# Layer 3 by Strassen's seven products over a pair of batches, in a float32r kernel of attention and two gated layers

## The reference, cut to what matters

```
x = attention(x, state)                        # 8 batches of 512 tokens and 32 states: rows of 512
x = ((x @ w1) * (x @ w2)) @ w3 @ w_out         # first stage, 4352 rows, d_ff 1024
h = x @ w_in                                   # second stage, layer 3: [rows, 512] @ [512, 2048]
g = h - tanh(h)
out = g @ w_out2                               # layer 4: [rows, 2048] @ [2048, 512]
```

## Time and profile before

| what | value |
|---|---|
| median of 3 runs | 1243.88 us (1243.76 to 1244.55) |
| profiled execution | span 1242.0 us, first to last instruction; the median of the runs is 1.9 us above it |
| TensorE (PE) | busy 1235.9 us, 6628 matmul records |
| VectorE (DVE), ScalarE (ACT) | busy 801.1 us (64%) and 547.7 us (44%) |
| DMA | 63.95 MB, mean 51 GB/s |
| stages | layer 3 begins at 492.6 us |

### The profile page before, as it was taken

The page is one execution under the profiler, slowest core; times in us unless marked ns, Lnnn a source line. Parts: engine busy times, 40 slices in busy tenths (PEclk is TensorE's granted clock), DMA queues, the critical chain, the costliest instruction groups (busy, mean ns, idle before and its releaser), DMA issues.

```text
span 1242.0 us, 16996 instructions
## 1 busy us (share of the span) xinstructions
PE 1235.9 (100%) x6628; PEld 1003.7 (81%) x6628; DVE 801.1 (64%) x1298; ACT 547.7 (44%) x1027; POOL 1.3 (0%) x7
## 2 busy tenths in 40 slices
PE   9999999999999999999999999999999999999998
PEld 6789777777777778888888888888888888888887
DVE  4666566555455435888677677676676776766776
ACT  6663334333333334545444444444444344444444
POOL 0000000000000000000000000000000000000000
PEclk9999999999999999999999999999999999999999
DMA  9932000000000120311101001001001001010000
GB/s 375 403 121 77 9 35 8 28 34 1 35 35 1 68 88 32 98 55 35 51 18 49 3 18 51 1 18 51 1 17 51 9 9 51 18 43 1 9 35 18
DMA packets 17786, 63.95 MB, mean 51 GB/s; under 512 B 1984, under 2 KB 3520, under 8 KB 13104
## 3 DMA queue, kind: packets, MB, share of 16 engines
q1 hardware_dynamic: 16976, 62.00, 13.7%
q10 hardware_dynamic: 704, 0.85, 0.2%
q0 software_dynamic: 32, 0.07, 0.0%
HBM read 45.09 MB, written 17.83 MB: 51 GB/s over the span
## 4 chain that ended last, share of the span: by engine, by line
issue 100%; POOLq 0%; POOL 0%
POOLq L261 0%; POOL ident L440 0%; POOL ident L438 0%; POOLq L440 0%; POOLq L1495 0%
## 5 line engine op out<-in xcount | busy, mean ns | idle before, releaser
L1273 ACT ACTIVATE hq<-bank 128x512 f32<-128x512 f32 (+1 forms) x144 | 82.7, 575 | 394.7 <-PE bank L1408 394.7
L1344 DVE TENSOR_TENSOR hw<-hw,hq 128x512 f32<-128x512 f32 (+1 forms) x144 | 95.5, 663 | 192.2 <-ACT hw L1284 191.9
L1408 PE MATMUL bank<-ysp_hi,wi_hi 128*128 128x512 f32 (+1 forms) x576 | 217.4, 377 | 0.0
L1408 PE MATMUL bank<-ysp_hi,wi_lo 128*128 128x512 f32 (+1 forms) x576 | 217.3, 377 | 0.0
L1408 PE MATMUL bank<-ysp_lo,wi_hi 128*128 128x512 f32 (+1 forms) x576 | 217.2, 377 | 0.0
L1435 PE MATMUL wide<-wz_hi,gsp_hi 128*128 128x512 f32 x544 | 212.3, 390 | 0.0
L1435 PE MATMUL wide<-wz_lo,gsp_hi 128*128 128x512 f32 x544 | 211.8, 389 | 0.0
L1435 PE MATMUL wide<-wz_hi,gsp_lo 128*128 128x512 f32 x544 | 211.7, 389 | 0.0
L1408 PEld LDWEIGHTS bank<-ysp_hi,wi_hi 128*128 128x128 f32 x576 | 108.3, 188 | 21.4 <-DVE gb L1363 0.9
L1408 PEld LDWEIGHTS bank<-ysp_lo,wi_hi 128*128 128x128 f32 x576 | 108.4, 188 | 20.4
L1408 PEld LDWEIGHTS bank<-ysp_hi,wi_lo 128*128 128x128 f32 x576 | 108.2, 188 | 19.9
(11 more groups left out here) (123 smaller groups left out, 1739.1 us busy)
## 6 DMA issues: line engine op xcount, KB each, us to landing
xT<-in_x_cols SPq DMA_DIRECT2D x8, 1024.0 KB, 8.6
xs<-in_x_rows SPq DMA_DIRECT2D x8, 1024.0 KB, 8.3
y_dram<-ysb SPq DMA_DIRECT2D x8, 1024.0 KB, 3.8
out<-ysb SPq DMA_DIRECT2D x8, 1024.0 KB, 4.6
yr<-y_dram SPq DMA_DIRECT2D x28, 256.0 KB, 4.1
w_raw<-in_moe_w SPq DMA_DIRECT2D x8, 512.0 KB, 10.8
wi_raw<-in_moe_w_in SPq DMA_DIRECT2D x4, 1024.0 KB, 7.6
raw<-in_moe_w_out SPq DMA_DIRECT2D x16, 256.0 KB, 2.6
```

Source lines behind the costliest of these rows:

```text
L1273: act.activation(hq[:, f % 2, 0:w], ph[f % 2][:, 0:w], ACT.Square).then_inc(sq_done, 1)
L1344: dve.tensor_tensor(u, u, q, ALU.mult).then_inc(w2_done, 1)
L1408: mm = pe.matmul(ph[f % 2][:, 0:w], wi[s][c][:, f * P:(f + 1) * P], ysp[k][u][c][:, 0:w], start=c + m == 0, stop=c == KC - 1 and m == LAST)
```

## The change

Only the second stage's first layer and what follows from it is changed; the front and the first stage's own layers compute as before.

**Seven products.** Two batches are taken together (pair i, tiles 2i and 2i+1), and two blocks of hidden columns (step p, 0 to 7). With w_in cut in four by inner half and by block (A11 to A22) and y cut in four by inner half and by batch (B11 to B22), the four blocks of h come from seven products in Winograd's form instead of eight. A product is 2 parts x 3 passes = 6 matmuls. Sums of A (S1 to S4) and of B (T1 to T4) are split into hi and lo like the blocks themselves. The products run in two PSUM banks, `acc` and `diff`, and three times an intermediate sum is copied out by ScalarE (`snap`) before the bank is gone on with.

**Weights by way of DRAM.** During the first stage `Pieces` loads w_in and w_out2, makes the four sums, splits everything and stores it to `wi_parts` and `wz_parts` in DRAM. In the second stage each step's seven split pieces (1.75 MB) are loaded anew into one of two slots, and each w_out2 block (0.5 MB) for each tile into one of six.

**Order.** In a step TensorE runs the seven products and, in four halves of 6 matmuls, two layer-4 blocks of the pair's first tile. g of the second tile (`g2`) is held in SBUF; its layer 4 runs after the eight steps, in `phase` and `other`, in the banks that the products used, and its last blocks go on into the next pair's step 0 (`column`). The states' tile runs inside that phase of the last pair, with w_in blocks from DRAM and without Strassen. The comparison `far` moves from VectorE to ScalarE (a Relu with a steep slope), and elementwise work is done 1024 wide, two blocks at once.

The core of the diff:

```diff
+    def load_wi(self, sp, n):
+        if n >= 2:
+            sp.wait_ge(self.p4_done, n - 1)
+            sp.wait_ge(self.p2_done, n - 1)
+        sp.dma_start(plain(self.wi[n % 2][:, :, :, :, :].rearrange("p s o k c -> p s o (k c)")), self.pieces.wi_parts[n % NP, :, :, 1:NOPS, :]
+                     ).then_inc(self.wi_in[n % 2], 16)
...
+    def product(self, pe, i, p, to, op, at, start, done):
+        n = NP * i + p
+        if p == 0:
+            pe.wait_ge(self.ysp_lo, NY * i + Y_ORDER.index(at) + 1)
+        wi = self.wi[n % 2]
+        for k in range(2):
+            for m, (s, t) in enumerate(PASSES):
+                mm = pe.matmul(to, wi[:, s, op - 1, k, :], (self.y_hi, self.y_lo)[t][:, at, k, :], start=start and k + m == 0,
+                               stop=k == 1 and m == LAST, skip_group_check=not start)
+        mm.then_inc(done, 1)
...
+    def p7(self, pe, i, p):
+        pe.wait_ge(self.su2_done, NP * i + p + 1)
+        self.product(pe, i, p, self.acc, S3, T3, False, self.p7_done)
...
+        def step(i, p):
+            n = NP * i + p
+            far2(n - 1)
+            if p == 1:
+                copy_s1(n)
+                copy_s5(n)
+            else:
+                copy_s5(n)
+                copy_s1(n)
+            high1(n - 1)
+            tanh2(n - 1)
+            copy_su2(n)
+            if p == NP - 1:
+                high2(i, 0)
+            square1(n)
+            far1(n)
+            tanh1(n)
+            copy_c21(n)
+            square2(n)
...
+        def first_step(i):
+            n = NP * i
+            add_c12(n)
+            if i == 0:
+                after_first(dve)
+            add_c22(n)
+            add_c11(n)
+        def step(i, p):
+            n = NP * i + p
+            poly1(n - 1, BOTH)
+            near1(n - 1, BOTH)
+            select1(n - 1, BOTH)
+            rest1(n - 1, BOTH)
+            poly2(n - 1)
+            low1(n - 1)
+            add_c12(n)
+            near2(n - 1)
+            add_c22(n)
+            select2(n - 1)
+            rest2(n - 1)
+            add_c11(n)
...
+        def first_step(i):
+            opening(i)
+            if i == 0:
+                finish(pe, range(2))
             else:
+                column(i - 1, 2, TAIL)
+            second.p6(pe, i, 0)
+            second.p3(pe, i, 0)
+            if i > 0:
+                column(i - 1, 3, TAIL[:2])
+            second.p7(pe, i, 0)
+            if i == 0:
+                finish(pe, range(2, KC))
             else:
+                column(i - 1, 3, TAIL[2:])
+            second.p4(pe, i, 0)
+            second.p2(pe, i, 0)
...
+        def step(i, p):
+            if p == 1:
+                second.p1(pe, i, p)
+                second.p5(pe, i, p)
+            else:
+                second.p5(pe, i, p)
+                second.p1(pe, i, p)
+                first(i, 2 * p - 3, 0)
+            second.p6(pe, i, p)
+            second.p3(pe, i, p)
+            if p > 1:
+                first(i, 2 * p - 3, 1)
+            second.p7(pe, i, p)
+            second.p2(pe, i, p)
+            first(i, 2 * p - 2, 0)
+            second.p4(pe, i, p)
+            first(i, 2 * p - 2, 1)
+        def phase(i):
+            first(i, 13)
+            for f in range(2):
+                block(i, 1, f, (0, 1))
+            first(i, 14)
+            first(i, 15)
+            for f in range(2):
+                block(i, 1, f, (2, 3)).then_inc(l4_second, 1)
...
+        for i in range(PAIRS):
+            at = 2 * NF2 * i
+            last = i == PAIRS - 1
+            for p in range(NP):
+                n = NP * i + p
+                load_wz(at + 2 * p + 3)
+                if n + 2 < NP * PAIRS:
+                    second.load_wi(sp, n + 2)
+                else:
+                    load_states_wi(n + 2 - NP * PAIRS)
+                if p == NP - 1 and not last:
+                    second.load_y(sp, i + 1)
+                load_wz(at + 2 * p + 4)
+                if p == 1 and i > 0:
+                    store_second(i - 1)
+            if not last:
+                load_wz(at + 19)
+                store_first(i)
+                for r in range(20, 2 * NF2 + 3):
+                    load_wz(at + r)
...
-                mm = pe.matmul(ph[f % 2][:, 0:w], wi[s][c][:, f * P:(f + 1) * P], ysp[k][u][c][:, 0:w],
-                               start=c + m == 0, stop=c == KC - 1 and m == LAST)
```

More of the change, by code:

```diff
@@ L74 @@
 WRING = 3
+NP = NF2 // 2
+NOPS = 8
+A21, A11, A12, A22, S1, S2, S3, S4 = range(NOPS)
+NY = 7
+B11, B21, B22, T1, T2, T3, T4 = range(NY)
+Y_ORDER = (T1, B11, T2, B22, T3, B21, T4)
+WZ = 6
+USES = [(0, f) for f in range(14)] + [(1, 0), (1, 1), (0, 14), (0, 15)] + [(1, f) for f in range(2, NF2)]
+NEAR, C3, C5 = 3.5 / 64, -1.0 / 3.0, 2.0 / 15.0
+ROOT = C5 ** 0.25
+KAPPA = C3 / C5 ** 0.5
+STEEP = 1e10
 class Map:
@@ L247, in build @@
-        y_hi, y_lo, y_out = sem("y2_hi"), sem("y2_lo"), sem("y_out")
-        y_copied = [sem("y_copied0"), sem("y_copied1")]
[L249 to L254, removed]
+        cut, cut_ready = small("cut", [P, 1]), sem("cut_ready")
+        l2_done, y_out = sem("l2_done"), sem("y_out")
@@ L258, in build @@
[L258 to L259 removed]
+                          w34, y_dram, s1_done, pieces, second, bank)
+        moe2 = stage_moe2(nc, sem, base, w_at, moe1["l1_done"], l2_done, y_copied, ys_out, y_out, second, pieces, y_dram, out, bank)
         with nc.Block("stages") as block:
@@ L1029, in entry, with layer2, tensor @@
                         rows.vector_back(dve, b + 2)
[L1030 to L1043 removed]
+                if not last:
+                    prepare(b, f)
+                elif f == 0:
+                    pieces.vector_half(dve, B - 1, 1)
+                elif f == 3:
+                    for n in (0, 1):
+                        second.vector_ysum(dve, 0, n)
+                elif f == 4:
+                    for n in (2, 3):
+                        second.vector_ysum(dve, 0, n)
+                elif f == 5:
+                    for n in (0, 1):
+                        second.vector_ysplit(dve, 0, n)
+                elif f == 6:
+                    for n in (2, 3):
+                        second.vector_ysplit(dve, 0, n)
+                elif f == 7:
+                    for n in (4, 5, 6):
+                        second.vector_ysplit(dve, 0, n)
+        for b in range(B):
+            entry(b, b % 2, last=b == B - 1)
+    def layer2(pe, b, f, cols=range(KC)):
+        n = NF1 * b + f
+        pe.wait_ge(p_lo, n + 1)
+        if f == 0:
+            if b == 0:
+                pe.wait_ge(ys_copied, KC)
+            for k in range(2):
+                after(pe, y_copied[k], 2 * b)
+        for c in cols:
+            for m, (s, t) in enumerate(PASSES):
+                mm = pe.matmul(py[c], w34[s][:, f, c * P:(c + 1) * P], psp[t][:, f % 2, :],
+                               start=f + m == 0, stop=f == NF1 - 1 and m == LAST)
+            if c == KC - 1:
+                mm.then_inc(l2_done, 1)
+    def tensor(pe):
         def layer1(b, f, k, last):
```

1215 lines of the change are left out of this document (827 added, 388 removed).

## The result

| | before | changed |
|---|---|---|
| median | 1243.82 us (1243.71 to 1244.55, 4 runs) | 1227.00 us (1225.78 to 1227.53, 4 runs) |
| profiled execution | span 1242.0 us | span 1223.9 us |

The ratio is 0.9862, 95% interval 0.985 to 0.9874: 16.8 us faster, where 23.2 were forecast (1220.7). In the profiled execution the granted clock was 1.00; in the other three runs it was 0.997 or 0.998 and the spans 1.0 to 1.8 us longer.

The account below looks back on a forecast made before the run. TensorE, fed all the time, was taken as the bound, so only fewer or faster matmuls help. -43.5 + 12.4 + 2.3 + 2.0 + 3.6 = -23.2: span 1242.0 to 1218.8, median 1220.7 us, range 1209 to 1240.

Parts of the forecast that it names:

- What goes: Layer 3 of the eight tiles: 192 of 1536 matmuls go, 0.227 us each, -43.5 us.
- A full step: Steps 2 to 7: VectorE's 12.8 us fit in TensorE's 14.96, P7 has 1.7 us to spare, nothing added.
- Step 1: Step 1 of each pair: TensorE stands 3.1 us at P6 and P7, four times, +12.4 us.
- Pair 0's P4: Pair 0, step 0: P4 waits for c22, which VectorE issues behind `after_first`, +2.3 us.
- Transition and transfers: Steps to phase: two level arrivals per pair, +2.0 us; second tile's block f = 4 late behind the store, +3.6 us.
- place (a): Loads at the end of the steps: landed at 26.5 at 407 GB/s, last needed at 28.6, priced 0.
- the rule: Trainium skill's HBM rate for one core, about 358 GB/s; by it place (a) lands at about 28.1, still in time.
- First stage: Work that `Pieces` adds to VectorE and ScalarE is covered by TensorE, 0; upper end +1.2 x 7.
- rival 1: Transfers late in every phase, by in-order queue waits or 322 GB/s or less: +8 to +20, 1229 to 1241; chance 0.14.
- rival 2: Hand-over chain before P7 decides every step: at +1.5 per step +36, 1257 us; chance 0.06.
- rival 3: Clock falls after step 1's waits: 30 matmuls per pair at 1.2 GHz, +24, 1245 us; chance 0.06.
- Rivals 4 (no change) and 5 (less would be paid): TensorE waits elsewhere, within 2.5 us of 1243.9, chance 0.04; step 1's waits half as long, late block hidden, 1211, chance 0.08.

Follow-up runs that it names:

- experiment 6: Changed kernel with product P7 done twice in steps 1 to 7 of each pair, 168 matmuls more: 1264.74 us.
- experiment 5: Changed kernel with two more 1024-column copies on ScalarE ahead of su2 in steps 3 to 7: 1239.21 us.
- experiment 2: Changed kernel with ScalarE's copies s1 and s5 ahead of far2, su2 right behind it, in step 1 of each pair: 1224.40 us.
- experiment 4: Changed kernel with VectorE's addition c22 of the very first step ahead of the copies of the last tile's y: 1223.60 us.
- experiment 1: Changed kernel with the second tile's w_out2 blocks f = 4 and 5 issued ahead of the 1 MB store, pairs 0 to 2: 1220.31 us.
- experiment 7: Changed kernel with the edits of experiments 1, 2 and 4 together: 1215.06 us.
- experiment 8: Changed kernel with experiments 1 and 4, experiment 3's order in step 1, and half w_out2 blocks ahead of P5 and P6 in step 2: 1212.88 us.
- experiment 3: Experiment 2 plus VectorE's order in step 1: c12 ahead of poly2 and low1, c22 right behind low1: 1230.78 us, changed kernel 1227.00.

## Why the prediction was right, and where it was off

The direction, the mechanism and the range (1209 to 1240) held; the time was 6.3 us too low. Of its four signs of being wrong two came, both in small: layer 3 starts at 493.4 us (the sign said later than 493), and the clock was under 1.00 in three of four executions. The other two did not: no full step is over 14.96 us, and releases by DMA add up to 6.5 us, not 10. By the steps of the prediction:

- **What goes, -43.5.** Right. 1344 matmuls, and 0.225 us for each that was added again (experiment 6).
- **A full step, 0.** Right: 14.96 us in every one. The spare in front of P7 was 1.4 us, not 1.7 (experiment 5).
- **Step 1, +12.4.** 13.8: 3.4 in pairs 1 to 3, where SyncE's loads over steps 1 and 2 are 29.20 us apart and the matmuls need 25.84, and 3.7 in pair 0, where two copies of y (L1108, 1.07 us) stand in ScalarE's queue ahead of them too. Cause right: moving the copies in ScalarE's queue moves the waits (experiment 2). Undersized by the spacing of dependent wide instructions on VectorE, 1.31 and 1.42 instead of 1.25 and 1.30.
- **Pair 0's P4, +2.3.** 2.25, and it goes with one line moved (experiment 4).
- **Transition and transfers, +2.0 and +3.6.** Together 10.4. This is the step that failed, in size. The late blocks cost 2.2 us and not 1.2 in each of three phases. Counted from the start of the last step (613.70 - 14.96 = 598.74) the store is issued at 30.0 and not 29.6, and the block is there at 36.4 and not 35.5: store and block one after the other take 6.4 us, not 5.9. Small waits add 0.5 a phase, as forecast. And the last pair's 2.1 us were not foreseen: 1.2 of them is the states' third layer 3, whose megabyte is only asked for when its buffer is free, at 1144.2, and is there 9.3 us later. For block f = 4 the rate was no part of it: the same bytes in the same window, four blocks of them ahead of the store, made no wait (experiment 1). But place (a), priced at 0, was not free. In pair 1 (last step from 768.10) block f = 2, issued ahead of the store and behind the pieces and the next y, was there after 29.4 us and not 26.5, and was due at 28.6. TensorE waited 0.6 for it. That made the phase no longer, since block f = 4 came no later for it; with f = 4's wait gone, 0.2 us in one phase stay (experiment 7). The first row below is of TensorE; the second is a window, with the DMA engines full (1.00):

```profile
797.60 1.63 PE L1981 MATMUL bank<-wz,gsp 128*128 128x512 f32 x6 [0.56 <-DMA wz<-wz_parts]
```

```profile
785.00:790.00 5.00, 5.00 (x23) 3.88 (x22) 4.93 (x7) 2.29 (x3) 0.00 (x0) 1.00 1.00 401
```

  The engines moved about the 407 GB/s that were taken; the sum let them start at 14.5 us, took 1 us for the last receipt, and left out the next block's 0.5 MB, issued 1.3 us behind. Which of the three made the 3 us, no run shows. (By the prediction's own terms the landing by the rule is 28.0, not 28.1.)
- **First stage, 0.** 0.5: layer 3's first matmul starts at 493.4 instead of 492.9.
- **The base.** Before had about 1.4 us of small waits of its own in its second stage (by the distances of matmul starts), which the sum had left in. They went with its code.

Sum: -43.5 + 13.8 + 2.25 + 10.4 + 0.5 - 1.4, and 0.1 at the end: -17.9, against 18.1 measured between the spans.

**The rivals.** Late transfers (rival 1) took part of the time, mostly by the queue's order; a wait of 0.6 us in pair 1 came with full DMA engines. The hand-over chain (rival 2) was 1.4 us from deciding. The falling clock (rival 3) was real and small: the forecast had 30 matmuls at 1.2 GHz in each step 1, +24 us. What comes is 3.4 us at the lower level, 1.7 us of time, behind some of the waits of 2 us; the 1.0 to 1.8 us by which three of the four runs of the changed kernel are longer fit about one such dip each, but those three have no trace. The Trainium skill (TensorE: Matmul & The Clock Gate, A second HAM failure mode) tells of a clock that goes up and down because TensorE idles briefly and often between groups of matmuls. The traces agree only in part: the clock does go down and up, but behind single waits of 1.8 to 2.2 us, while twenty new waits of 0.2 us (experiment 5) and eight of up to 0.8 (experiment 8) brought no dip of their own. Where the two halves of step 1's wait became one (experiment 3) the dips cost more than the edit gained. Rivals 4 (no change) and 5 (less would be paid) fell.

What stays open: why a wait of 2 us is followed by a dip in one phase and not in the next (in the profiled execution of the changed kernel, with waits of up to 2.2 us, none was), and where the 0.5 us of the first stage go. That these waits bring the dips is shown by where the dips stand and by which kernels have them; how, no run shows.

## What to carry to other kernels

When a change takes work off the bounding engine, price what is left by the queues: list, for each wait of that engine, what stands ahead of the releasing instruction on its own engine, because that order, more than the amount of work, set most of the time lost here, and a few lines moved brought back 18 us. Take the spacing of dependent instructions from the trace per kind and not one figure for all, and ask at each link whether another engine holds it up: 0.8 us of spacings and one wait of 0.5 made a joint cost 2.9 us instead of 1.7. And count a wait of 2 us on TensorE as up to 3.7: where it can't be removed, cover half of it, since in the profiled executions the clock stayed up behind every wait of less than 1.8 us.

## What the runs showed of the hardware

- A dip of the granted clock behind a wait of 1.8 to 2.2 us begins 0.1 to 1.5 us after TensorE resumes and lasts 3.4 us at half speed, 1.7 us of lost time: all eleven seen in five kernels have this size. Two of them (experiments 5 and 6) hid a wait that came next, and cost 0.3. Each stands behind such a wait, but only 11 of the 38 such waits in the profiled executions have one; behind the some 60 of 0.7 to 1.8 us there is none.
- `copy_predicated` of 1024 columns takes 1.32 us, and the next dependent instruction starts 1.34 to 1.42 after its start; for the other wide VectorE instructions (1.22 us) it is 1.25 to 1.36.
- A 512 KB load issued 0.4 us behind a 1 MB store took 6.0 us to land, 1.9 us too late; issued ahead of the store it caused no wait (experiment 1).
